# Turning gathered rows with VectorE's 32x32 transposes instead of TensorE in a mixture-of-experts stage

## What is computed

```
attn:  q, k, v (2, 8, 768, 64); window 128, 4 sinks; softmax; a @ v
dense: x (1536, 512); h = x @ w_in (512, 2048); g = h - tanh(h); y = g @ w_out
moe:   x = y; logits = x @ w_gate; noise_scale = log1p(exp(x @ w_noise))
       noisy = logits + noise_scale * noise; top 2 of 8; weights = softmax of the two
for e in range(8):
    h = maximum(x[mask] @ w1[e], 0)          # w1[e] (512, 1024)
    out[mask] += weight * (h @ w2[e])        # w2[e] (1024, 512)
```

## Time and profile before

| | us |
|---|---|
| median of 3 runs | 745.41 (744.26 to 745.78) |
| the profiled execution | 744.54 |
| its span, first to last instruction | 742.8 |
| TensorE busy | 729.9 |
| VectorE busy | 355.3 |
| ScalarE busy | 230.0 |
| GpSimd busy | 451.0 |

### The profile page before, as it was taken

The page is one execution under the profiler, slowest core; times in us unless marked ns, Lnnn a source line. Parts: engine busy times, 40 slices in busy tenths (PEclk is TensorE's granted clock), DMA queues, the critical chain, the costliest instruction groups (busy, mean ns, idle before and its releaser), DMA issues.

```text
span 742.8 us, 12879 instructions
## 1 busy us (share of the span) xinstructions
PE 729.9 (98%) x3892; PEld 617.5 (83%) x3893; DVE 355.3 (48%) x883; ACT 230.0 (31%) x529; POOL 451.0 (61%) x252
## 2 busy tenths in 40 slices
PE   7999999999999999999999899999999999999998
PEld 6677889999899898998887788888888888888886
DVE  4777554233523442344456554454544544544544
ACT  5999632223223322232241221122112211211212
POOL 6888999000300030005969996948986898887774
PEclk9999999999999999999999999999999999999999
DMA  8742376000200020005363567867786778767776
GB/s 273 274 144 95 109 276 246 0 1 1 86 0 1 0 85 0 0 0 198 110 257 128 191 210 253 265 212 239 247 269 209 236 264 267 246 211 228 246 239 222
DMA packets 59551, 121.46 MB, mean 164 GB/s; under 512 B 7040, under 2 KB 21504, under 8 KB 59520
## 3 DMA queue, kind: packets, MB, share of 16 engines
q1 hardware_dynamic: 28512, 63.92, 25.3%
q10 hardware_dynamic: 27168, 44.57, 17.9%
q0 software_dynamic: 3840, 12.59, 5.1%
HBM read 81.74 MB, written 39.32 MB: 163 GB/s over the span
## 4 chain that ended last, share of the span: by engine, by line
PE 97%; ACT 1%; DVE 1%; POOL 1%; issue 0%; POOLq 0%; ACTq 0%; DVEq 0%
PE bank L1652 23%; PE bank L1620 23%; PE bank L1477 18%; PE bank L1527 18%; PE bank L1430 4%; PE bank L1421 3%; PE bank L1403 3%; PE bank L1602 2%; PE bank L1543 1%; PE bank L1537 1%; ACT arena L789 1%; PE bank L1486 1%; POOL arena L686 0%; DVE hid L1222 0%; PE bank L1630 0%
## 5 line engine op out<-in xcount | busy, mean ns | idle before, releaser
L664 POOL TENSOR_TENSOR ring<-ring_raw,ring 128x2048 fp32r<-128x2048 f32 x32 | 148.2, 4630 | 2.5
L710 POOL DMA_INDIRECT sorted_x<-y_rows,arena x24 | 24.6, 1026 | 205.9 <-DVEq L1158 199.8
L1652 PE MATMUL bank<-ring,hidT_hi 128*128 (+1 forms) x464 | 145.9, 395 | 1.4 <-DVE hidT_lo L1235 1.0
L662 POOL TENSOR_TENSOR ring<-ring_raw,ones 128x2048 fp32r<-128x2048 f32 x32 | 115.9, 3623 | 41.7 <-DMA ring_raw<-in_moe_w 41.6
L1620 PE MATMUL bank<-ring,xsT_hi 128*128 (+1 forms) x496 | 133.3, 390 | 2.3 <-DVE hid L1222 2.0
L1527 PE MATMUL bank<-w_out_sb,gated_hi 128*128 128x512 f32 x384 | 121.2, 397 | 0.0
L1620 PEld LDWEIGHTS bank<-ring,xsT_hi 128*128 128x128 f32 x496 | 92.7, 188 | 22.3 <-issue 3.3
L1652 PEld LDWEIGHTS bank<-ring,hidT_hi 128*128 128x128 f32 x464 | 85.0, 188 | 18.2 <-issue 1.8
L1652 PE MATMUL bank<-ring,hidT_lo 128*128 (+1 forms) x232 | 90.7, 391 | 0.0
L1077 DVE TENSOR_TENSOR arena<-bank,arena 128x384 f32<-128x384 f32 x64 | 35.7, 557 | 113.8 <-ACT arena L844 112.9
L1477 PE MATMUL bank<-xT_hi,w_in_hi 128*128 (+1 forms) x256 | 87.0, 340 | 0.0
(11 more groups left out here) (203 smaller groups left out, 1078.8 us busy)
## 6 DMA issues: line engine op xcount, KB each, us to landing
ring_raw<-in_moe_w SPq DMA_DIRECT2D x48, 512.0 KB, 4.1
hid_by_lane<-hid ACTq DMA_DIRECT2D x28, 512.0 KB, 3.5
hid_lanes<-hid_by_lane ACTq DMA_DIRECT2D x28, 512.0 KB, 4.7
ring_raw<-in_moe_w SPq DMA_DIRECT2D x8, 1024.0 KB, 6.4
sorted_y<-ys ACTq DMA_DIRECT2D x31, 256.0 KB, 2.5
xs<-sorted_x ACTq DMA_DIRECT2D x27, 256.0 KB, 3.4
sorted_y<-zeros SPq DMA_DIRECT2D x1, 4864.0 KB, 25.9
arena<-in_k SPq DMA_DIRECT2D x8, 520.0 KB, 4.0
```

What stands on the lines that cost most here:

```text
L662: pool.tensor_tensor(hi, raw, one_like(raw), ALU.mult).then_inc(rounded, 1)
L664: ins = pool.tensor_tensor(lo, raw, hi.bitcast(F32), ALU.subtract)
L1652: last = pe.matmul(bank[5 + b][:, :], x[:, c * P:(c + 1) * P], ring[:, bass.ds(at * 2 * WE + (w + CH * FE + c * DM), DM)], start=c == 0 an ...
```

## The change

From tile 5 on, the gathered rows come with four DMAs in place of one. DMA b loads columns 128 b to 128 b + 127 of the 128 rows into the 32 partitions from 32 b on: partition 32 b + i gets them of rows 4 i to 4 i + 3, so that `sorted_x` is read in pieces of 512 bytes. VectorE then turns `xs` with one instruction of 32x32 transposes into `bank[0]`, ahead of relu_out(t) in each pass, and the four TensorE transposes of tiles 5 to 30 go. After such a turn, partition 32 b + r of chunk c holds input 128 b + 4 r + c, which is 4 times the partition plus c. The first matrix's loads are changed to this order for all experts (partition p, chunk c holds row 4 p + c), and the TensorE turns that stay (tiles 0 to 4) read columns with a stride of four. The load's wait and the reading of the tile's row are as before.

```diff
+    LANE = P // QUAD
+        xs_cols = xs[:, :].rearrange("p (r c) -> p c r", c=CH)
+        xs_lanes = xs[:, :].rearrange("p (g q) -> p g q", g=QUAD)
+        xs_blocks = xs[:, :].rearrange("p (g r c) -> p g c r", g=QUAD, c=CH)
...
-        w1_view = w1.rearrange("e (c p) f -> p (e c) f", p=P)
+        w1_view = w1.rearrange("e (p c) f -> (e p) c f", p=P)
...
-                src = w1_view[:, bass.ds(expert * CH + j * (CH // 2), CH // 2), :]
+                src = w1_view[bass.ds(expert * P, P), j * (CH // 2):(j + 1) * (CH // 2), :]
...
+            def load_lanes(t):
+
+                act.wait_ge(xs_turned, t)
+                at = act.value_load(tile_row_i[0:1, bass.ds(t, 1)], min_val=0, max_val=E * CAP - P)
+                for b in range(QUAD):
+                    act.dma_start(xs_lanes[b * LANE:(b + 1) * LANE, :, :],
+                                  sorted_x[bass.ds(at, P), b * P:(b + 1) * P].rearrange("(i g) q -> i g q", g=QUAD)
+                                  ).then_inc(lanes_loaded, 16)
...
             rows_turned_out(4)
-            load_rows(5)
+            load_lanes(5)
             hid_in(2, first=True)
...
                 rows_turned_out(t + 1)
-                load_rows(t + 2)
+                load_lanes(t + 2)
                 hid_turned_out(t - 1, used=t)
...
+            def turn_lanes(t):
+
+                dve.wait_ge(lanes_loaded, 16 * QUAD * (t - 4))
+                dve.wait_ge(xsT_ready, t)
+                dve.transpose(bank[0][:, :].rearrange("p (c i g) -> p g c i", c=CH, g=QUAD),
+                              xs_blocks).then_inc(xs_turned, 1)
...
             def tile(t):
+                turn_lanes(t + 1)
                 relu_out(t, written=True)
...
+            turn_lanes(TILES - 1)
             relu_out(TILES - 2, written=True)
...
-                    last = pe.transpose(bank[0][:, c * P:(c + 1) * P], xs[:, c * P:(c + 1) * P], ident[:, :])
+                    last = pe.transpose(bank[0][:, c * P:(c + 1) * P], xs_cols[:, c, :], ident[:, :])
...
             with pe.Fori(4, TILES - 2) as t:
                 up(t, evicted=True)
-                turn_rows(t + 1)
                 down(t - 2)
             up(TILES - 2, evicted=True)
-            turn_rows(TILES - 1)
```

More of the change, by code:

```diff
@@ L416, in build @@
         xs_loaded = sem("xs_loaded")
+        lanes_loaded = sem("lanes_loaded")
         hid_written = sem("hid_written")
```

## The result

The changed kernel took 750.22 us (median of 6 runs, 748.51 to 754.22) against 744.84 us for the kernel before (6 runs beside it, 744.11 to 747.17). The ratio is 1.0078, with a 95% interval of 1.0049 to 1.0108. The profiled execution took 750.34 us with a span of 748.6 us. The forecast was 738.4 us in a range of 733 to 743, so both its size and its sign were wrong. Nearly every step on the turn itself came as described. Two steps failed: the new order of the first matrix, costed at nothing, and the start of the steady stage, costed at 1.2 us.

A forecast was written before the change was run, and what follows sets the result against it. TensorE, 98% busy, bounds the kernel; afterwards GpSimd's 742.1 - 9.5 + 1.2 + 20 x 0.1 = 735.8 ends behind TensorE's 733.1. Adding 1.74 and 0.87 gives 738.4 us, range 733.0 to 743.0.

The forecast's parts named there:

- the start of the steady stage: Entry to the loop: three more issues delay hid_in(2) and down(2), then VectorE's new turn; 1.2 us, bounds 0 to 2.5.
- The turn's 0.49 us: Between up and down on TensorE: each removed turn of four transposes saves 0.49 us, 26 times, 12.7 us.
- the tile of 10.88: Steady expert stage on TensorE: a tile takes 10.88 us without its turn, instead of 11.37.
- 512-byte pieces priced nearly by their bytes: Row loads on ScalarE's queue: 512 packets of 512 B take what 128 of 2 KB do, about 24 ns each.
- rival 3: Where the turn was: down's register loads and waits show, leaving 0.13 of 0.49 us per turn; 743.2 us; chance 0.05.
- rival 4: VectorE's new turn: lanes landing later than 6.0 us after issue set the tile; at 7.0 us, 759 us; chance 0.07.
- SP's hold: Weight loads: SP, held by down(14) until 569.00, is released 6.4 us earlier, and the last loads and gathers move with it.
- GpSimd's side ending last: Gathers at the end: 742.1 - 9.5 + 1.2 + 20 x 0.1 = 735.8 us, later than TensorE, so it sets the span.
- the first matrix costs nothing: First matrix's loads and strided turns: still one 4 KB row per partition, only the row differs; nothing, bounds 0 to 0.5 us.
- d: Weight loads: how much slower one half-piece load gets; 0.1 us, bounds 0 to 0.7, counted 8 to 36 times.
- TensorE's side: TensorE's span: 742.8 - 12.7 + 1.2 + 1.0 + 8 x 0.1 = 733.1 us, the 1.0 a wait at up(21).
- Rival 2: Transfer engines fill up: a tile's 512 packets cost 46 ns each, weight loads slow by 0.7 us; 758.3 us; chance 0.12.

The follow-up runs named there:

- host_rows: The changed kernel with the first matrix laid out on the host in its order of use and read as the kernel before reads it: 742.36 us, ratio 0.9943.
- host_six: The changed kernel with lane loads starting at tile 6 and the first matrix laid out on the host in order of use: 742.83 us, ratio 0.9943.
- host_late: The changed kernel with the first matrix laid out on the host and load_lanes(5) moved behind hid_in(2) and relu_out(3): 745.14 us, ratio 0.9976.
- from_six: The changed kernel with lane loads starting at tile 6, tile 5 keeping the plain load and TensorE's turn, nothing on the host: 750.69 us, ratio 1.0047.

## Why the prediction was wrong, step by step

**Right.** The turn's 0.49 us and the tile of 10.88; VectorE's 26 turns of 1.1 us beside other work; 512-byte pieces priced nearly by their bytes (0.182 x 748.6 - 0.179 x 742.8 is some 3 us of 16 engines more in all, 0.1 per tile); no hole where the turn had been (rival 3); lanes that land in 3.4 us in the median, so that VectorE's idle time ahead of its new turn sums to 12.6 us and TensorE doesn't wait for it in the steady tile (rival 4); SP's hold as the thing that sets when the last loads go out; GpSimd's side ending last.

**Failed: "the first matrix costs nothing".** The step said that a half piece stays one 4 KB row per partition and only the row differs, and priced that at 0 to 0.5 in all. It compared the shape of the transfer and not the distance between its rows. The order costs 0.8 us on each first-matrix step of the changed kernel (0.7 with the order alone). The forecast's d, the slowdown of a half-piece load, was 0.1; it came out at 4.82 - 4.54 = 0.28 over the 35 steps. It agrees with the first matrix alone: 16 x 0.80 = 12.8, less four steps from one expert to the next that shrank from 6.24 to 5.64, is 10.4, and 35 x 0.28 is 9.8.

The Trainium skill (DMA: Bandwidth & Descriptors, section Latency and other measured facts) has copies between HBM tensors slow down where the partitions' rows lie a large power of two apart (207 GB/s at 512 KiB, 103 at 4 MiB, 214 at 4 MiB with a pad of 4 KiB), and recommends a pad of a few KiB. The runs agree with the remedy (4 KB of pad brought the step from 4.8 back to 4.2 us), here at a distance of 16 KB.

**Mis-sized: the start.** Its term was 1.2 us, bounds 0 to 2.5. The step followed the delay to down(2), 0.6 us, and put the rest of the 1.2 on VectorE's new turn. It put `hid_in(2)` off by 1.5 us (2.6 measured) and didn't follow its landing on: `hid_out(3)`, `hid_in(3)`, `hid_out(4)` and so up(5) hang on it, three landings in a row, which also took 3.3 us longer than before. Cost at up(5): 5.9 us, and some 2 more for the lower clock right behind it.

**How they add up.** The forecast put the last load at 655.08 - 6.4 + 1.2 + 2.0 = 651.9; it went out at 663.94, 12.0 later. The hold at down(7), six turns into the gain, should have ended at 489.50 - 2.9 + 1.2 = 487.8 and ended at 495.24, 7.4 later. From there 35 steps at 0.28 instead of 0.1 are 6.3 more. The forecast had 1.7 in hand ahead of its hold at down(14) (487.8 + 35 x 4.64 = 650.2, against 651.9), which was used up: 7.4 + 6.3 - 1.7 = 12.0. The gathers stand behind those loads: the first was forecast at 668.26 - 3.2 = 665.1 and came at 677.18, 12.1 later. The end is 12.8 later than forecast; the last gather landed 2.1 slower and the last store 1.5 faster than taken. So on GpSimd's side nearly all of the miss passes through the load chain, and the late start is most of its first 7.4 us.

TensorE's side is as late. It would have ended near 743.11 + 3.56 = 746.7 (an estimate from its last copy and the kernel before's), 13.6 over its 733.1: 5.9 - 1.2 = 4.7 for the start, 1.8 ahead of the stage, 4.4 for the two slow ups and 4.67 - 1.8 = 2.9 for the hole, 13.8 in all. The sum had no term for a lower clock after a hole.

**Rivals.** Rival 2 had the effect (slower, from d = 0.34 on in its sum, loads spaced over 4.5 us) with the wrong cause: it blamed the packets of `sorted_x`. Against that stand the queue's 18.2% and `host_rows`, with the same packets and loads 4.54 us apart; the 4.80 of `host_six` leaves a smaller share of it open. With the late start beside it a d of 0.28 was enough. Its chance of 0.12 was for one cause of slower loads only; that loads could slow for another reason had no case at all, and this is where the 0.15 for slower was too low. The sum did name what mattered: GpSimd's side was 0.7 us from being the bound, and every extra tenth of a microsecond on a load counts 20 to 36 times there.

**Still open.** Why 16 KB is a bad distance for 4 KB pieces; why 64 partitions with 8 KB each are worse still; why loads in the old order took 4.6 to 4.8 us in `host_late` and `host_six`; why the transfers of the start took longer; why the kernel before loses 0.2% with pairs.

## What to carry to other kernels

When a weight layout is permuted to suit another operation, price the load again by the distance between its rows, not only by their size; where rows end up a power of two apart, try a pad. Where an engine's queue issues DMAs for others, follow each landing behind an inserted issue to the last one who waits. When taking work off the busiest engine, look for the serial chain just behind it: here one load in flight at a time capped the gain, and with a pair in flight the ratio went from 0.9943 to 0.9892 (two intervals that overlap a little).

## What the runs showed of the chip that I had not expected

- A 512 KB load of 128 rows of 4 KB took 4.2 us per step with its rows 4 KB apart (in the kernel before and in `host_rows`; 4.6 in `host_late` and `host_six`) or 4.3 with them 20 KB apart (padded), and 4.9 to 5.2 us with them 16 KB apart. The loads of the second matrix, read the same way everywhere, took 4.4 to 4.8.
- 512-byte pieces cost little more than their bytes: at equal bytes, 11232 packets more raised the queue's share of 16 engines from 17.9% to 18.2%.
- An issue by ScalarE took 0.36 us for the plain row load and 0.57 to 0.73 us for a lane load. The forecast had about 0.5 for it.
- After holes of 2.6 to 5.6 us TensorE's next 24 matmuls took 7.1 to 8.1 us instead of 5.44 (7.35 after 2.71 and 7.90 after 4.67 in the changed kernel, 7.06 after 3.90 in `host_late`, 8.10 after 5.59 in `from_six`), with one exception: after 2.79 us in `host_late` they took 5.76. In the changed kernel the granted clock was 0.91 and 0.92 over the stretches with the two of them, between its levels of 1.2 and 2.4 GHz. After holes of 1.37 and 1.74 us the up took 5.70 and 5.73.
- A TensorE transpose of 128x128 whose input columns lie four apart loaded its weights in 208 ns in the median, with adjacent columns in 139; a tile with four of them took 11.41 us instead of 11.36.
- Two 512 KB loads in flight together took 5.8 to 8.3 us for the pair, against some 9 for one after the other.
